# Seven weight loads of a fused attention and soft-MoE kernel, joined into three loads with longer rows

## What is computed

```python
kv = einsum('bhsd,bhse->bhde', k, v)              # 8 batches, 8 heads, 576 tokens, width 64
o = einsum('bhsd,bhde->bhse', q, kv)
x = (o / sqrt(mean(o * o, -1) + 1e-6) * g_norm)   # then reshaped to [4608 tokens, 512]
logits = x @ phi                                  # 32 slots: 8 experts with 4 slots each
d = softmax over the 4608 tokens of logits
slot_input = d.T @ x                              # [8 experts, 4 slots, 512]
slot_out[e] = relu(slot_input[e] @ w1[e]) @ w2[e] # w1: 8 x 512 x 1024, w2: 8 x 1024 x 512
out = softmax over the 32 slots of logits @ slot_out
```

## Time and profile before

| | before |
|---|---|
| median of 3 runs | 172.0 us (171.95 to 172.03) |
| the profiled execution | 172.08 us |
| its span, first to last instruction | 170.8 us |
| mean granted TensorE clock | 0.973 of full speed |
| TensorE busy (matmul; weight load) | 148.7 us (87%); 104.9 us (61%) |
| DVE, ACT, POOL busy | 86.5 (51%), 89.0 (52%), 59.6 us (35%) |
| moved by the DMA engines | 71.65 MB |

### The profile page before, as it was taken

How to read it: one execution, slowest core, us unless ns; L and a number is a source line. 1 busy time by engine, 2 the same in 40 slices (tenths; PEclk the granted TensorE clock), 3 DMA queues, 4 the chain that set the end, 5 groups by cost and what they waited for, 6 DMA issues and landing times.

```text
span 170.8 us, 4238 instructions
## 1 busy us (share of the span) xinstructions
PE 148.7 (87%) x1832; PEld 104.9 (61%) x1832; DVE 86.5 (51%) x185; ACT 89.0 (52%) x230; POOL 59.6 (35%) x73
## 2 busy tenths in 40 slices
PE   7887897989999899999899998989999989989300
PEld 3466776979678888896697674346655543455000
DVE  1122156283677265762936698824888137218300
ACT  3127576786975887869759864202224046217400
POOL 7000708548357755367482679400000004000000
PEclk9999999999999999999999999999999999999955
DMA  5999999999999999999999999999999999999996
GB/s 188 420 425 425 441 423 436 478 415 473 427 414 408 470 427 432 403 418 432 430 434 430 426 413 422 436 445 405 434 430 434 457 422 393 425 424 426 432 452 259
DMA packets 4365, 71.65 MB, mean 420 GB/s; under 512 B 790, under 2 KB 790, under 8 KB 922
## 3 DMA queue, kind: packets, MB, share of 16 engines
q1 hardware_dynamic: 3994, 71.18, 97.7%
q0 software_dynamic: 352, 0.20, 0.4%
HBM read 61.94 MB, written 9.44 MB: 418 GB/s over the span
## 4 chain that ended last, share of the span: by engine, by line
PE 58%; DMA 13%; ACT 12%; DVE 7%; SPq 2%; issue 1%
PE psum L93 58%; DMA arena<-in_kv_dram 13%; ACT bd L93 3%; ACT sq L93 3%; ACT xall L93 2%; SPq L93 2%; DVE logits L93 1%; DVE arena L93 1%; ACT arena L93 1%; DVE ms L93 1%; ACT part L93 1%; ACT d L93 1%; DVE part L93 1%; ACT r L93 1%; DVE acc L93 1%
## 5 line engine op out<-in xcount | busy, mean ns | idle before, releaser
L93 PE MATMUL psum<-bd,arena 128*128 128x192 f32 (+1 forms) x320 | 56.1, 335 | 2.0 <-ACT bd L93 1.6
L93 PEld LDWEIGHTS psum<-bd,arena 128*128 128x128 f32 (+1 forms) x320 | 45.4, 179 | 8.7 <-ACT bd L93 3.8
L93 DVE TENSOR_REDUCE ms<-sq 128x16 f32<-128x1024 f32 (+1 forms) x19 | 22.1, 1162 | 32.7 <-ACT sq L93 32.4
L93 POOL TENSOR_TENSOR part<-part,r 128x512 f32<-128x512 f32 x17 | 17.8, 1048 | 49.5 <-DVE r L93 49.5
L93 POOL TENSOR_TENSOR xall<-xall,r 128x512 f32<-128x512 f32 x34 | 34.7, 1042 | 0.0
L93 ACT ACTIVATE sq<-psum 128x512 f32<-128x512 f32 x36 | 21.5, 598 | 12.7 <-PE psum L93 12.5
L93 PE MATMUL psum<-arena 128*64 128x64 f32 (+1 forms) x640 | 21.7, 226 | 3.0 <-DMA arena<-in_kv_dram 2.5
L93 PEld LDWEIGHTS psum<-arena 128*64 128x64 f32 (+1 forms) x640 | 19.0, 137 | 8.4 <-DMA arena<-in_kv_dram 3.7
L93 ACT COPY xall<-psum 128x512 f32<-128x512 f32 x34 | 20.6, 606 | 0.0
L93 ACT COPY part<-psum 128x256 f32<-128x256 f32 (+1 forms) x38 | 13.6, 359 | 11.2 <-DVE part L93 10.1
L93 DVE TENSOR_REDUCE logits<-part 128x64 f32<-128x512 f32 (+1 forms) x18 | 17.8, 990 | 0.0
(11 more groups left out here) (80 smaller groups left out, 123.5 us busy)
## 6 DMA issues: line engine op xcount, KB each, us to landing
arena<-in_w_dram SPq DMA_DIRECT2D x4, 4096.0 KB, 23.4
arena<-in_w_dram SPq DMA_DIRECT2D x4, 2048.0 KB, 20.1
arena<-in_t_dram SPq DMA_DIRECT2D x1, 6912.0 KB, 36.2
arena<-in_w_dram SPq DMA_DIRECT2D x2, 3072.0 KB, 22.7
arena<-in_kv_dram SPq DMA_DIRECT2D x2, 2304.0 KB, 23.5
arena<-in_kv_dram SPq DMA_DIRECT2D x1, 4608.0 KB, 42.7
arena<-in_kv_dram SPq DMA_DIRECT2D x1, 3584.0 KB, 32.3
arena<-in_kv_dram SPq DMA_DIRECT2D x3, 1152.0 KB, 13.4
```

The lines of the kernel that those rows point to most:

```text
L93: self.inst, self.token = method(*args, **kwargs), None
```

## The change

The seven early weight loads become three, with rows of 63, 63 and 50 KB (`W_LOADS`). The weights are listed in blocks of 1 KB (`EARLY_W`), and a row may start and end in the middle of a unit. The x buffers become the end of the arena, so that the third row runs from block 126 through the arena's end into them. Homes of k, v, q and output chunks move. The first joined load is issued after T = 18 and waits for `o_made[17]`, the second after T = 27 and waits for `kvs[7].read`, the third after the loop and waits for `summed`. Batch 7's steps move to T = 26, 27, 28. In the expert stage the order of `expert_h` and `expert_y` changes, and the last load (w2 unit 7) waits for `h_read[4]` and is issued after `expert_h(4)`. The bytes moved and the arithmetic stay.

```diff
-KV_AT = (0, 36, 54, 0, 90, 126, 18, 54)
-Q_AT = (18, 72, 108, 36)
-W_AT = {
...
-W_ROWS = (
...
+KV_AT = (0, 106, 124, 0, 52, 70, 106, 124)
+Q_AT = (142, 34, 88, 142)
+def blocks(*units):
+    return [(kind, u, lo + i) for kind, u, lo, n in units for i in range(n)]
+EARLY_W = blocks(
+    ("w1", 0, 0, 16), ("w1", 1, 0, 16), ("w2", 0, 0, 16), ("w2", 1, 0, 16), ("w2", 2, 8, 8), ("w1", 2, 0, 16),
+    ("w1", 3, 0, 16), ("w1", 4, 0, 16), ("w1", 5, 0, 16), ("w2", 2, 0, 8), ("w1", 6, 0, 16), ("w1", 7, 0, 16),
+)
+W_LOADS = (
+    (0, EARLY_W[:63]), (63, EARLY_W[63:126]), (126, EARLY_W[126:]),
+    (0, blocks(("w2", 3, 0, 16))), (16, blocks(("w2", 4, 0, 16))),
+    (72, blocks(("w2", 5, 0, 16), ("w2", 6, 0, 16))), (104, blocks(("w2", 7, 0, 16))),
+)
-OUT_AT = tuple(range(72, 144, 6))
+OUT_AT = tuple(range(0, 72, 6))
...
-    arena = sbuf([P, HEAD + ARENA], F32, "arena")
+    arena = sbuf([P, HEAD + ARENA + NX * 4 * 129], F32, "arena")
-    xall = sbuf([P, NX, 4, 129], F32, "xall")
+    xall = shaped(arena[:, HEAD + ARENA :], [P, NX, 4, 129])
...
+    def load_w(j, after):
+        at, row = W_LOADS[j]
+        lo = sum(len(r) for _, r in W_LOADS[:j]) * KB * P
+        n = len(row) * KB
+        src = w_in[:, lo : lo + n * P].rearrange("o (p n) -> (o p) n", p=P)
+        landed = dma(sp, place(at, n), src, after)
+        for i, block in enumerate(row):
+            w_home[block], w_landed[block] = place(at + i, KB), landed
...
     kv_steps.update({(6, i - 4): (i,) for i in range(3)})
-    del kv_steps[6, -1]
+    kv_steps.update({(7, i - 5): (i,) for i in range(3)})
+    for late in ((6, -1), (7, -2), (7, -1)):
+        del kv_steps[late]
...
-        18: lambda: load_w("w1", 0, after=[o_made[17]]),
-        21: lambda: load_w("w2", 0, after=[kvs[5].read]),
-        24: lambda: load_w("w1", 2, after=[kvs[6].read]),
-        27: lambda: load_w("w1", 4, after=[o_made[26]]),
-        30: lambda: load_w("w1", 5, after=[kvs[7].read]),
+        18: lambda: load_w(0, [o_made[17]]),
+        27: lambda: load_w(1, [kvs[7].read]),
...
-    load_w("w2", 2, 0, after=[o_made[Z]])
-    load_w("w1", 7, after=[summed])
+    load_w(2, [summed])
...
     expert_h(0)
-    load_w("w2", 3, after=[h_read[0]])
+    load_w(3, [h_read[0]])
     expert_h(1)
-    load_w("w2", 4, after=[h_read[1]])
+    load_w(4, [h_read[1]])
     expert_y(0, 0)
     combine(0)
     expert_h(2)
     expert_y(1, 0)
     combine(1)
-    for e in range(3, NE):
-        expert_h(e)
-        if e == 3:
-            load_w("w2", 5, after=[h_read[3]])
-        if e == 4:
-            combine(2)
-        if e == 5:
-            load_w("w2", 7, after=[h_read[5]])
+    expert_h(3)
+    load_w(5, [h_read[3]])
+    expert_h(4)
+    load_w(6, [h_read[4]])
+    combine(2)
+    expert_y(0, 1)
+    expert_y(1, 1)
+    expert_h(5)
+    expert_h(6)
     expert_y(2, 0)
     expert_y(3, 0)
-    expert_y(0, 1)
-    expert_y(1, 1)
+    expert_h(7)
     for e in range(4, NE):
         y_made = expert_y(e, 0)
```

More of the change, by code:

```diff
@@ L32 @@
 LATE = 6
-KV_AT = (0, 36, 54, 0, 90, 126, 18, 54)
-Q_AT = (18, 72, 108, 36)
-W_AT = {
[3 rows of a table removed]
-}
-W_ROWS = (
[L41 to L51, removed]
-)
-OUT_AT = tuple(range(72, 144, 6))
+KV_AT = (0, 106, 124, 0, 52, 70, 106, 124)
[5 more added lines that the diff above has]
+    ("w1", 3, 0, 16), ("w1", 4, 0, 16), ("w1", 5, 0, 16), ("w2", 2, 0, 8), ("w1", 6, 0, 16), ("w1", 7, 0, 16),
+)
+W_LOADS = (
[4 more added lines that the diff above has]
+OUT_AT = tuple(range(0, 72, 6))
 OUT_ROWS = ((0, 1, 2), (3, 4, 5), (6, 7), (8, 9, 10, 11))
@@ L121, in shaped @@
     return t[:, : int(np.prod(shape[1:]))].rearrange(f"p ({dims}) -> p {dims}", **{f"d{i}": n for i, n in enumerate(shape[1:])})
-def row_length(row):
-    return sum(UNIT if part is None else UNIT // 2 for _, _, part in row)
 def first_pieces(out):
@@ L165, in soft_moe_linear_attention @@
     banks = nc.alloc_psum_tensor("psum", [P, 8 * 512], F32).ap().rearrange("p (b n) -> p b n", n=512)
-    arena = sbuf([P, HEAD + ARENA], F32, "arena")
+    arena = sbuf([P, HEAD + ARENA + NX * 4 * 129], F32, "arena")
     phi_sb = arena[:, :128].rearrange("p (g w n) -> p g w n", g=2, w=2)
     g2 = arena[:, 128:129]
-    xall = sbuf([P, NX, 4, 129], F32, "xall")
-    xflat = xall.rearrange("p i j n -> p (i j n)")
+    xall = shaped(arena[:, HEAD + ARENA :], [P, NX, 4, 129])
     def place(at, n):
@@ L187, in q_rest @@
         return place(Q_AT[g], TOK)[:, 4096:].rearrange("p (i r n) -> p i r n", i=2, r=NPAIR)
[L189 to L205, removed]
+    w_home, w_landed = {}, {}
+    def load_w(j, after):
[6 more added lines that the diff above has]
+            w_home[block], w_landed[block] = place(at + i, KB), landed
     def w_block(kind, u, i):
[L209 to L212, removed]
+        return w_home[kind, u, i], w_landed[kind, u, i]
     def load_row(at, src, after=()):
@@ L764, in soft_moe_linear_attention @@
     q_landed[1, 1] = kv_landed[4, 0] = kv_landed[4, 1] = load_row(Q_AT[1] + 8, kv4_in)
-    q_landed[2, 0] = q_landed[2, 1] = kv_landed[5, 0] = kv_landed[5, 1] = load_row(Q_AT[2], kv5_in)
+    q_landed[2, 0] = q_landed[2, 1] = kv_landed[5, 0] = kv_landed[5, 1] = load_row(KV_AT[5], kv5_in)
     def load_t3():
@@ L1205 @@
     kv = kv.reshape(B, P, TOK)
-    w = {("w1", e, None): w1[e] for e in range(NE)} | {("w2", u, None): w2[u] for u in range(NE)}
-    w |= {("w2", 2, i): w2[2][:, i * UNIT // 2 : (i + 1) * UNIT // 2] for i in range(2)}
-    rows = [np.concatenate([w[k] for k in row], axis=1).reshape(-1) for row in W_ROWS]
+    w = {"w1": w1.reshape(NE, P, 16, KB), "w2": w2.reshape(NE, P, 16, KB)}
+    rows = [np.concatenate([w[kind][u, :, i] for kind, u, i in row], axis=1).reshape(-1) for _, row in W_LOADS]
     first = np.zeros((P, HEAD + 2304), np.float32)
@@ L1217 @@
         "in_kv4_dram": np.concatenate([qm[1][:, 2048:], kv[4]], axis=1),
-        "in_kv5_dram": np.concatenate([qm[2], kv[5]], axis=1),
-        "in_t3_dram": np.concatenate([kv[6], qm[3], kv[7]], axis=1),
+        "in_kv5_dram": np.concatenate([kv[5], qm[2]], axis=1),
+        "in_t3_dram": np.concatenate([kv[6], kv[7], qm[3]], axis=1),
         "in_w_dram": np.concatenate(rows)[None],
```

## The result

The changed kernel takes 172.97 us (median of 7 runs, 172.53 to 173.70) where the kernel before takes 171.95 beside it: a ratio of 1.0063, with a 95% interval of 1.0047 to 1.0079. It is slower by about 1 us, and its runs scatter by 1.2 us where those of before scatter by 0.3. The forecast was no change, 171.8.

The account below looks back on a forecast made before the run. A DMA transfer stream that never stops was taken to set the end. From the profiled 172.08 us, four loads fewer gave -0.2, all else 0: 171.88, and the median lies 0.08 lower, 171.8 us; range 171.3 to 172.3.

Parts of the forecast that it names:

- the waits on SP: SP's joined loads after the first: each issued in time before the one ahead runs dry, 0 us.
- Rival A: SP's wait for `summed`: the third joined load comes late, an average engine stands 0.7 us, 172.5 us; chance 0.10.
- The uneven ends: DMA engines at the end: one that fetches or stores more may end last, up to 0.3 us either way, 0.08.
- Four loads fewer: DMA stream: same bytes, 36 packets fewer on each of 16 engines, -0.2 us.
- Rival B: DMA loads: the fixed price is larger, -0.35 to -0.8 us, so 171.2 to 171.65; chance 0.26.
- Batch 7 and the experts: TensorE: 0.5 us wait at step 0 replaces 0.62 for `top`; `expert_h(5)` starts at 126.1 without waiting; 0 us each.
- Room at the end: Last store: PE may be about 0.8 us late at the end before the end moves.
- Rivals C and D: C: instruction fetches wait behind long rows, 176 us, chance 0.02; D: each load pays its own start, 162 us, 0.01.

Follow-up runs that it names:

- experiment 1: The changed kernel run again with no edit, for a second trace: 173.71 us, ratio 1.0092.
- experiment 8: Experiment 2's kernel with batch 7's steps back where the kernel before has them, so the second joined load goes out at 88.30: 175.09 us, ratio 1.0187.
- the first trace: The trace of the changed kernel from its first measurement, before it was run again: traced run 172.97 us.
- experiment 2: The changed kernel with its third joined load in two, 34 blocks issued after the last product, 16 after `summed`: 171.77 us, ratio 0.9994.
- experiment 4: The changed kernel with two matmuls on zeros put ahead of `expert_y(6, 0)`, where TensorE waits for w2 unit 4: 173.71 us, ratio 1.0104.
- experiment 5: Experiment 2's kernel with the second joined load held back to the last product of tile 27, issued at 85.66: 173.30 us, ratio 1.0077.
- experiment 6: The kernel before, short rows and seven loads kept, its sixth early load held back to the end of the fill matmuls: 173.87 us, ratio 1.0120.

## Why the prediction was wrong

**The step that failed** is the one on the waits on SP: "with 2.5 us it flows at 107.1, 1.1 us ahead. 0 us." Both of its numbers were wrong. The 2.5 us, taken from the kernel's first load as what lies at both ends of a transfer, were meant as an upper bound. Leads of 1.7 to 2.1 us cost 1.0 to 1.8 us in the medians, one of 2.8 cost 0.2, which its interval cannot tell from nothing, and at 3.1 and 3.2 none was seen. And the 1.1 us were counted for an average engine, from how unevenly the engines end at the kernel's end. At load 2 they are further apart: the first is done with load 1 at 106.63 and the last at 109.81, and it is the first ones that stand. A wait of the stream is reckoned from the first engine that runs dry, not from the landing, which tells of the last. That alone would not have given the loss: an estimate with 2.5 us and the sixteen ends of load 1 in the trace has an average engine stand for 0.13 us, where load 2 cost it 0.4 (0.8 in experiment 1). To give these, the 2.5 would have to be 3.3 and 3.7. Why a load close behind another costs more than one that meets idle engines (2.2 us, experiment 8) stays open.

The Trainium skill (DMA: Bandwidth & Descriptors, Latency and other measured facts) gives a first byte after some 600 ns on this kind of queue. By that figure, as an estimate, a lead of 1.7 us would be ample. The runs do not agree: on idle engines the first rows began 0.95 us after the issue at the earliest and ran long (experiment 8), and with leads of 1.7 to 1.9 us the stream was held up all the same. The measurement decides.

**Rival A** had the place (load 2), the mechanism and the sign. It made the loss hang on `summed` coming after 105.7, though; `summed` came at 104.7, as before, and the loss was there. Its chance of 0.10 went with that condition. Of its two signs neither showed: the DMA line has no dip near 107 us. Its price of 0.7 us was about what an average engine loses (0.4 in the first trace, 0.8 in experiment 1). The uneven ends, which the forecast had at up to 0.3 us either way, added as much again in experiment 1, and in the first trace the late last store came on top.

**Four loads fewer, -0.2 us:** the packets fell as counted. The kernels with three loads fewer and no stop came out 0.1 us faster, within their intervals; a term of that size fits, and 0 does too. Rival B has nothing for it.

**Batch 7 and the experts, 0 us each:** right, instruction by instruction (0.52 us for 0.62, 126.19 for 126.1), and experiment 2 bears the sum out. The forecast also saw what the early steps are for, but sized it too small: for a load 1 issued at 88.2 it had the stream stop for 1.2 us, and experiment 8, with 88.30, shows 2.0 us on an average engine and 3.2 us in the time.

**Room at the end, 0.8 us:** on the small side. In the first trace the last store went out 2.3 us later than before and landed 0.9 us later, at 171.58: 1.9 us at both ends of it instead of 2.5 make the room 1.4 us.

**Rivals C and D:** no wait of TensorE without a named cause appeared between 70 and 125 us, and no gain of several microseconds. Nothing speaks for either.

## What to carry to other kernels

In a kernel like this one, where a stream of transfers sets the time, joining loads takes issues away, and each issue left must come earlier. Find for every load the first engine's end of the load ahead, and keep some 3 us between the issue and that; where a joined load waits for its latest part, issue the rest without it. A landing row tells when the last engine is through, so the lead it suggests is too long by the spread of the engines, here 3 us.

## What the runs showed of the hardware that was not expected

TensorE's granted clock fell to half (1.2 of 2.4 GHz) for 3.4 us at 147 to 148 us in the traces of the changed kernel, of experiment 4 and of experiment 5, and not in the others. The changed kernel, stretches of TensorE's time ahead of and in the fall (us, PE, PEld, DVE, ACT, POOL, PEclk, DMA share, GB/s):

```profile
139.00:147.00 8.00, 7.15 (x48) 3.03 (x44) 5.16 (x6) 4.70 (x6) 1.73 (x3) 1.00 0.98 417
147.00:150.50 3.50, 3.50 (x33) 1.58 (x36) 0.00 (x0) 0.48 (x1) 0.00 (x0) 0.52 1.03 429
```

The same kernel in experiment 1:

```profile
139.00:147.00 8.00, 7.15 (x51) 2.98 (x43) 5.16 (x6) 4.70 (x6) 1.73 (x3) 1.00 0.97 414
147.00:150.50 3.50, 3.50 (x69) 2.13 (x72) 0.00 (x0) 0.48 (x1) 0.00 (x0) 1.00 1.04 431
```

TensorE was busy for the same 7.15 of 8 us ahead of it in both. The wait at 135 us does not set it off by itself: it was filled in experiment 4, where the clock fell, and 2.38 us long in experiment 6, where it did not. What does is left open. Its price is read from these two traces of one kernel: 7.05 against 5.39 us for the same 96 instructions, and a last store 1.85 us later, of which 0.17 were there ahead of the fall (147.16 against 146.99).

A store met engines that had run dry more gently than a load: the changed kernel's last store was issued at 162.48, its rows began at 163.31, 0.8 us later, on fifteen of the sixteen engines within 0.2 us of each other, and the first of them took the 0.9 us that the others took. Experiment 8's load 1 needed 0.95 to 1.47 us, and its first rows ran longer by 0.4 to 1.0 us. Why is left open.
